# A causal seven-tap convolution ahead of two dense layers: part of the first tiles' taps moved from VectorE to TensorE as matmuls with diagonal matrices

## The reference, cut to what matters

```python
# x: (2, 4096, 192); weight: (8, 7); w_in: (192, 2048); w_out: (2048, 192), for both layers
w = softmax(weight, axis=-1)                                  # 8 heads of 24 channels, 7 taps
y[b, s, c] = sum_k w[head(c), k] * x_pad[b, s + k, c]         # causal: six zeros ahead of x
x = y.reshape(8192, 192)
h = x @ w_in1
P = a0 + a1*h + a2*h**2 + a3*h**3
Q = 1 + |b0|*|h| + |b1|*h**2
x = (P / (Q + 1e-6)) @ w_out1                                 # first layer: rational
h = x @ w_in2
out = (s * max(h, 0)**2 + b) @ w_out2                         # second layer: squared ReLU
```

## Time and profile before

| what | us |
|---|---|
| median of 3 runs | 1335.89 (1335.84 to 1336.78) |
| the profiled execution: its own time | 1336.83 |
| the profiled execution: span of its records | 1335.0 |
| PE busy | 1259.8 (94% of the span) |
| DVE busy | 1160.5 (87%) |
| ACT busy | 1098.3 (82%) |
| POOL busy | 333.9 (25%) |

### The profile page before, as it was taken

How to read it: one execution, slowest core, us unless ns; L and a number is a source line. 1 busy time by engine, 2 the same in 40 slices (tenths; PEclk the granted TensorE clock), 3 DMA queues, 4 the chain that set the end, 5 groups by cost and what they waited for, 6 DMA issues and landing times.

```text
span 1335.0 us, 16225 instructions
## 1 busy us (share of the span) xinstructions
PE 1259.8 (94%) x5920; PEld 1069.3 (80%) x5920; DVE 1160.5 (87%) x1073; ACT 1098.3 (82%) x1053; POOL 333.9 (25%) x145
## 2 busy tenths in 40 slices
PE   3665899999999999999999999999999999999998
PEld 2544688888888888888888888888888888888887
DVE  7999999998899989999899989999899998978810
ACT  4766788888888888888888888888898888888833
POOL 4233222222222222222222222222222222222200
PEclk9787899999999999999999999999999999999999
DMA  5310100001000100001000010001000000000000
GB/s 134 103 32 0 24 1 12 1 1 36 0 12 0 36 0 0 12 0 36 0 12 0 0 36 0 12 0 36 0 0 12 0 12 1 13 1 13 0 13 12
DMA packets 17885, 20.40 MB, mean 15 GB/s; under 512 B 1472, under 2 KB 13760, under 8 KB 17600
## 3 DMA queue, kind: packets, MB, share of 16 engines
q1 hardware_dynamic: 17712, 20.00, 5.5%
q10 hardware_dynamic: 144, 0.01, 0.0%
HBM read 13.72 MB, written 6.29 MB: 15 GB/s over the span
## 4 chain that ended last, share of the span: by engine, by line
PE 75%; DVE 12%; ACT 6%; issue 5%; POOL 0%; DVEq 0%; ACTq 0%
PE o L340 22%; PE h L314 7%; PE h L317 7%; PE h L315 7%; PE h L316 7%; PE h L318 7%; PE o_tail L329 3%; PE o L327 3%; PE o L328 3%; PE o_tail L331 3%; PE o L330 3%; DVE work L610 3%; DVE work L651 2%; DVE work L649 1%; DVE work L612 1%
## 5 line engine op out<-in xcount | busy, mean ns | idle before, releaser
L297 POOL TENSOR_TENSOR gl<-work,gh 128x1024 fp32r<-128x1024 f32 x128 | 309.1, 2415 | 913.2 <-ACT gh L477 913.2
L340 PE MATMUL o<-v,work 128*128 128x192 f32 x2048 | 355.8, 327 | 3.4 <-ACT work L492 3.4
L340 PEld LDWEIGHTS o<-v,work 128*128 128x128 f32 x2048 | 338.2, 190 | 20.9 <-ACT work L492 11.2
L314 PE MATMUL h<-x_hi,w_hi 128*128 128x512 f32 x512 | 226.5, 442 | 61.5 <-DVE work L615 40.6
L610 DVE SCALAR_TENSOR_TENSOR work<-work,coef,h 128x1024 f32<-128x1024 f32 x128 | 163.6, 1278 | 91.9 <-ACT work L470 91.9
L317 PE MATMUL h<-x_tail,w_tail_hi 128*128 128x512 f32 x512 | 206.6, 403 | 0.0
L315 PE MATMUL h<-x_lo,w_hi 128*128 128x512 f32 x512 | 206.3, 403 | 0.0
L468 ACT ACTIVATE work<-h,coef 128x1024 f32<-128x1024 f32 x128 | 153.9, 1203 | 63.2 <-PE h L318 58.1
L316 PE MATMUL h<-x_hi,w_lo 128*128 128x512 f32 x512 | 205.8, 402 | 0.0
L318 PE MATMUL h<-x_tail,w_tail_lo 128*128 128x512 f32 x512 | 204.6, 400 | 0.0
L480 ACT ACTIVATE work<-work 128x1024 f32<-128x1024 f32 x128 | 135.9, 1062 | 65.7 <-DVE work L610 63.9
(11 more groups left out here) (62 smaller groups left out, 1563.2 us busy)
## 6 DMA issues: line engine op xcount, KB each, us to landing
out_dram<-y_out SPq DMA_DIRECT2D x16, 384.0 KB, 2.6
xt<-in_x_main_dram SPq DMA_DIRECT2D x7, 518.0 KB, 4.7
xt_tail<-in_x_tail_dram SPq DMA_DIRECT2D x8, 259.0 KB, 5.4
work<-in_moe_w_out_dram SPq DMA_DIRECT2D x1, 1536.0 KB, 10.9
v<-in_moe_w_out_dram SPq DMA_DIRECT2D x1, 1536.0 KB, 7.2
work<-in_moe_w_in_dram SPq DMA_DIRECT2D x1, 1024.0 KB, 9.3
work<-in_moe_w_in_dram SPq DMA_DIRECT2D x2, 512.0 KB, 5.6
xt<-in_x_main_dram SPq DMA_DIRECT2D x2, 259.0 KB, 4.9
```

Of the source, the lines that this page charges most:

```text
L297: nc.gpsimd.tensor_tensor(gl[:, j % 2, :], r_buf[j % 2], gh[:, j % 2, :].bitcast(F32), ALU.subtract).then_inc(gl_ready, 1)
L314: pe.matmul(h[:, half, :], hi[:, c], x_hi[:, :], start=True, stop=False)
L340: last = pe.matmul(o2[:, c // 2, c % 2, 0:D], g, v2[:, f, :], start=(f == 0 and c % 2 == 0), stop=(f == FT - 1), skip_group_check=True)
```

## The change

Four of the first tile's seven main taps, all of the second tile's, and all of the second pair's (main channels of both batches and the tail) become matmuls on PE. Each tap is one full fp32 matmul of 512 columns with a 128x128 matrix that has the tap's weights on its diagonal, accumulated in a PSUM bank of `o2` that isn't used yet. POOL makes an identity, ACT scales it by a column of `cw` into the diagonals (seven for the main channels, seven more for the tail in the same memory later). ACT copies finished convolutions to SBUF (`copy_of_conv`) for tiles 1 to 3 and the tail; for the first tile DVE adds PE's part to its own three taps. ACT does tap 0 of the first tail. `CONV_AT` says in which unit PE takes which taps, always between its product for unit n + 1 and its second product for unit n - 3. The column sum goes from unit 4 to unit 3. `load_x(1)` waits for PE's second-tile taps in place of DVE's. w_out1 and w_out2 are laid out on the host by partition, so that each partition reads one run of 12 KB, and w_out1 is loaded ahead of the coefficients. Later pairs stay on DVE by `TAPS_AT`.

```diff
-    TAPS_AT_FIRST = {(0, 0): (("second", 0), ("second", 1)), (0, 1): (("second", 2), ("second", 3)),
-                     (0, 2): (("second", 4), ("second", 5)), (0, 3): (("second", 6),),
-                     (0, 6): (("pair", 0), ("tail", 0)), (0, 7): (("pair", 1), ("tail", 1)),
-                     (1, 0): (("pair", 2), ("tail", 2)), (1, 1): (("pair", 3), ("tail", 3)),
-                     (1, 3): (("pair", 4), ("tail", 4)), (1, 4): (("pair", 5), ("tail", 5)),
-                     (1, 5): (("pair", 6), ("tail", 6))}
+    PE_TAPS_OF_FIRST = (3, 4, 5, 6)
+    DVE_TAPS_OF_FIRST = (0, 1, 2)
+    CONV_AT = {0: (("second", (0, 1)),), 1: (("second", (2, 3)),), 2: (("second", (4, 5, 6)),),
+               4: (("pair_a", (0, 1, 2)),), 5: (("pair_a", (3, 4, 5)),),
+               6: (("pair_a", (6,)), ("pair_b", (0, 1))), 7: (("pair_b", (2, 3, 4)),), 8: (("pair_b", (5, 6)),),
+               10: (("tail", (0, 1, 2)),), 11: (("tail", (3, 4, 5, 6)),)}
...
+            sp.dma_start(raw_v1, w_out1).then_inc(v1_loaded, 16)
...
-                sp.wait_ge(main_step, counted(main_taps(pair - 1)))
-                sp.wait_ge(tail_step, counted(pair * TAPS))
+                sp.wait_ge(conv_summed, 2 if isinstance(pair, int) and pair == 1 else 5)
+                sp.wait_ge(tail_step, counted(tail_steps(pair - 1)))
...
+            nc.gpsimd.memset(ident, 0.0).then_inc(ident_ready, 1)
+            pool.wait_ge(ident_ready, 1)
+            nc.gpsimd.affine_select(out=ident, in_=ident, compare_op=ALU.not_equal, fill=1.0, base=0,
+                                    pattern=[[-1, P]], channel_multiplier=1).then_inc(ident_ready, 1)
...
+            def conv_taps(bank, rows, taps, first, last):
+                for k in taps:
+                    done = pe.matmul(conv_bank[bank], diag[k], rows[:, k:k + TOK], start=(k == first),
+                                     stop=(k == last))
+                if taps[-1] == last:
+                    done.then_inc(conv_summed, 1)
...
+                    if group == "tail":
+                        if starts:
+                            pe.wait_ge(diag_ready, 2 * TAPS)
+                            pe.wait_ge(conv_copied, 2)
+                        conv_taps(1, xt_tail[:, :], taps, 0, TAPS - 1)
...
+            pe.wait_ge(x0_loaded, 32)
+            for i, k in enumerate(PE_TAPS_OF_FIRST):
+                pe.wait_ge(diag_ready, i + 1)
+                conv_taps(0, xt[:, 0, :], (k,), PE_TAPS_OF_FIRST[0], PE_TAPS_OF_FIRST[-1])
...
-                    if j == 4 and first(t):
+                    if j == 3 and first(t):
...
+                    if early:
+                        conv_of_unit(n)
...
+            def diagonal(k, rows):
+                nc.scalar.activation(diag[k], ident, ACT.Identity, scale=cw[:, rows, k:k + 1]).then_inc(diag_ready, 1)
+            def copy_of_conv(dst, bank):
+                nc.scalar.copy(dst, conv_bank[bank]).then_inc(conv_copied, 1)
...
+            for k in PE_TAPS_OF_FIRST:
+                diagonal(k, 0)
+            act.wait_ge(x0_loaded, 32)
+            nc.scalar.activation(conv_tail[:, :], xt_tail[:, 0:TOK], ACT.Identity,
+                                 scale=cw[:, 1, 0:1]).then_inc(tail_step, 1)
             high_of_w1(0)
+            for k in DVE_TAPS_OF_FIRST:
+                diagonal(k, 0)
...
+                    if first(t) and j == 3:
+                        act.wait_ge(conv_summed, 2)
+                        copy_of_conv(conv[:, 1, :], 1)
+                    if first(t) and j == 7:
+                        act.wait_ge(conv_summed, 3)
+                        act.wait_ge(x1_lo_ready, 2)
+                        copy_of_conv(conv[:, 0, :], 1)
+                    if second(t) and j == 1:
+                        act.wait_ge(conv_summed, 4)
+                        for k in range(TAPS):
+                            diagonal(k, 1)
+                        act.wait_ge(x1_lo_ready, 4)
+                        copy_of_conv(conv[:, 1, :], 0)
+                    if second(t) and j == 4:
+                        act.wait_ge(conv_summed, 5)
+                        copy_of_conv(conv_tail[:, :], 1)
...
-            for k in range(TAPS):
+            for k in DVE_TAPS_OF_FIRST:
                 main_tap(slice(0, 1), k, 0, k)
-            for k in range(TAPS):
-                tail_tap(k, 0)
+            for k in range(1, TAPS):
+                tail_tap(k, 0, k)
+            dve.wait_ge(conv_summed, 1)
+            dve.wait_ge(main_step, len(DVE_TAPS_OF_FIRST))
+            nc.vector.tensor_tensor(conv[:, 0, :], conv_bank[0], conv[:, 0, :], ALU.add).then_inc(main_step, 1)
...
-                    if first(t) and j == 5:
+                    if first(t) and j == 4:
                         dve.wait_ge(colsum_ready, 1)
```

More of the change, by code:

```diff
@@ L130, in conv_rational_relu2_kernel @@
         y_out = sb("y_out", [P, SUB, D])
-        ones = y_out[:, 0, 0:P]
+        y_flat = y_out[:, :, :].rearrange("p c d -> p (c d)")
+        ones = y_flat[:, 0:P]
+        diag_more = sb("diag_more", [P, 3, P])
+        diag = [y_flat[:, (k + 1) * P:(k + 2) * P] for k in range(5)] + [diag_more[:, k, :] for k in range(2)]
+        ident = diag_more[:, 2, :]
         bias_row = sb("bias_row", [P, D])
@@ L146, in conv_rational_relu2_kernel @@
         o2 = psum("o2", [P, 2, 2, 256])
+        conv_bank = [o2[:, bank, :, :].rearrange("p a b -> p (a b)") for bank in range(2)]
         h1_flat = h1[:, :, :].rearrange("p a b -> p (a b)")
@@ L256, in phase @@
                     sp.wait_ge(w_lo_ready, 8)
[L257 removed]
+                    sp.dma_start(v2[:, :, :], w_out2).then_inc(v2_loaded, 16)
                     sp.wait_ge(v1_lo_ready, 2)
@@ L343, in second_product_2, with conv_of_unit @@
                 last.then_inc(out2_done, 1)
+            def conv_taps(bank, rows, taps, first, last):
[4 more added lines that the diff above has]
+                    done.then_inc(conv_summed, 1)
+            def conv_of_unit(n):
+                for group, taps in CONV_AT.get(n, ()):
+                    starts = taps[0] == 0
+                    if group == "second":
+                        if starts:
+                            pe.wait_ge(diag_ready, TAPS)
+                            pe.wait_ge(x0_second_loaded, 16)
+                        conv_taps(1, xt[:, 1, :], taps, 0, TAPS - 1)
+                    if group == "pair_a":
+                        if starts:
+                            pe.wait_ge(conv_copied, 1)
+                            pe.wait_ge(x_loaded, 32)
+                        conv_taps(1, xt[:, 0, :], taps, 0, TAPS - 1)
+                    if group == "pair_b":
+                        if starts:
+                            pe.wait_ge(bias_row_ready, 1)
+                        conv_taps(0, xt[:, 1, :], taps, 0, TAPS - 1)
+                    if group == "tail":
+                        if starts:
+                            pe.wait_ge(diag_ready, 2 * TAPS)
[5 more added lines that the diff above has]
+                conv_taps(0, xt[:, 0, :], (k,), PE_TAPS_OF_FIRST[0], PE_TAPS_OF_FIRST[-1])
             def product_of_layer_1(n, j, t, parity):
@@ L522, in tail_tap @@
                 else:
-                    dve.wait_ge(tail_step, counted(pair * TAPS + k))
+                    dve.wait_ge(tail_step, counted(step))
                     ins = nc.vector.scalar_tensor_tensor(dst, x_k, w_k, dst, ALU.mult, ALU.add)
@@ L530, in split_conv @@
                 done = pair * 2 + batch
-                dve.wait_ge(main_step, counted(TAPS if isinstance(done, int) and done == 0 else main_taps(pair)))
-                dve.wait_ge(tail_step, counted((pair + 1) * TAPS))
+                if isinstance(done, int) and done == 1:
+                    dve.wait_ge(conv_copied, 1)
+                else:
+                    dve.wait_ge(main_step, counted(main_steps(pair)))
+                    dve.wait_ge(tail_step, counted(tail_steps(pair)))
+                    if not isinstance(pair, int) or pair > 0:
+                        dve.wait_ge(conv_copied, 4)
                 dve.wait_ge(h1_ready, counted((done - 1) * UNITS))
@@ L634, in phase @@
                         split_conv(i, 1)
-                    for what, k in at(i, TAPS_AT, TAPS_AT_FIRST).get((parity, j), ()) if tile(t) else ():
-                        if what == "second":
-                            if k == 0:
-                                dve.wait_ge(x0_second_loaded, 16)
-                            main_tap(slice(1, 2), k, 0, TAPS + k)
-                        elif pair_exists(i + 1):
-                            if what == "pair":
-                                main_tap(slice(0, 2), k, i + 1, main_taps(i) + k)
-                            else:
-                                tail_tap(k, i + 1)
+                    convolves = tile(t) and pair_exists(i + 1) and not (first(t) or second(t))
+                    for what, k in TAPS_AT.get((parity, j), ()) if convolves else ():
+                        if what == "pair":
```

(6 more changed lines are left out.)

22 lines of the change are left out of this document (14 added, 8 removed).

## The result

The changed kernel takes 1320.64 us (median of four, 1320.41 to 1321.37) against 1335.87 for the kernel before: a ratio of 0.9886, 95% interval 0.9868 to 0.9903. The forecast was 1321.0, 14.8 us of gain against 15.2 of the medians. In the two profiled executions the span went from 1335.0 to 1319.0 us.

What follows compares the result with a forecast made beforehand. DVE was taken to bound the start (units 1 to 11) and TensorE the unchanged steady part. The terms 4.3 + 11.9 + 0.6 - 1.0 - 1.0 gave 14.8 us of gain, 1321.0 us against the median, range 1315 to 1328.

Steps and rivals of the forecast that it cites:

- part 1: Before unit 0: sharing the first tile's taps starts the first product earlier, gaining 4.3 us (3.0 to 5.3).
- part 2: Unit 0: no gain, since its two second-tile taps lie beside ACT's four casts, which set the chain.
- part 3: Units 1 to 11: taking pure tap time off DVE gains 11.9 us, with units left at 7.4 or so.
- part 5: TensorE's and ACT's new work: low-clock restarts make products late in units 4 (0.3) and 10 (0.7), -1.0 us (0 to -4.5).
- the two ends: Before unit 0: the first product's length, 2.4 us at full clock and 4.7 at the low clock.
- Part 4: POOL's subtractions beside DVE: unit 8 gains a net 0.6 us more, unit 9 gains 1.0 less than first counted.
- The rule that was quoted: Unit 9: two-SBUF-input VectorE and SBUF-reading GpSimd instructions exclude one another, first to issue goes first; sum 1.7 us less.
- warm rival: Start and unit 13: TensorE's clock doesn't fall with more matmuls between waits; gain about 19 us, 1317; chance 0.12.
- second rival: Units 4, 5 and 9: POOL and TensorE lag, unit 9 at 12.2 us; gain 9, total 1327; chance 0.20.
- slower rival: Units 2 to 11: TensorE at the low clock becomes the bound, 21 us slower, 1357; chance 0.05.
- The head start alone: Only the gain before unit 0 counts, as the ACT chain needs what DVE gave up: 4.3 us, 1331.5; chance 0.03.

Runs made afterwards that it cites:

- the combined kernel: Tail diagonals made early, POOL's second subtraction moved later and TensorE's first-tile taps repeated before the first product, all against the changed kernel: median 1317.62 us.

## Why the prediction was right

By its own terms, in us of gain, from the table of units:

| term | forecast | measured |
|---|---|---|
| part 1, before unit 0 | 4.3 | 3.3 |
| part 2, unit 0 | 0 | 0.1 |
| part 3, units 1, 2, 3, 6, 7, 11 | 8.1 | 8.3 |
| units 8 (parts 3 and 4) | 2.5 | 2.5 |
| unit 9 (parts 3 and 4) | 0.9 | 0.0 |
| unit 5 | 0 | 0.3 |
| part 5, units 4 and 10 | -1.0 | 0.0 |
| units 12 and 13 | 0 | 1.4 |
| sum | 14.8 | 15.9 |

**What bounds the start.** Right: DVE. Every unit without other work (1, 2, 3, 6, 7, 11) fell to 7.41 to 7.43, the 7.4 that was read off, and the chain through ACT did not take over. The steady units did not move.

**Part 1.** Right in its mechanism, short by 1.0. The split ended 0.2 us later than worked out; and the product took 4.2 us, not the 3.4 that lay between the two ends. Its price was sized wrongly, and the run with the repeated taps shows that the clock was the cause. The idle time it was read from was wrong too: TensorE's four taps took 5.4 us, not 6.9, so it stood idle for 4.36 us ahead of the product and not for 3.0. Taps that were faster than forecast, while DVE was the later one, were of no use and made the gap longer. Nor would 3.0 us have been safe: with the old layout the product began at the low clock behind 3.03 us, and in the run with nine more matmuls behind 2.93. A full fp32 tap at the high clock took 0.87 to 0.89 us as forecast.

**The layout.** Right: nothing, with 0.4 us as the most. The run gave 0.17 in the trace.

**Part 3.** Right to 0.2 us over six units. **Part 4.** Unit 8 right. Unit 9 is the term that was mis-sized: it took 11.44, between the 9.5 of one stretch and the 12.2 of two, and I had taken 10.5, nearer to one. Both stretches came. The rule that was quoted (the Trainium skill, SBUF — State Buffer, Who interferes with whom) was the better guide: each operation of DVE with two SBUF inputs that met a running subtraction waited for its end. The 12.2 overshot since a wait is 2.0 us, not a whole 2.4. Two runs show the mechanism: either edit that takes one meeting away takes 2.0 us off the unit, both together 4.0.

**Part 5.** Its lateness of TensorE did not show in units 4 and 10. For unit 10 the mechanism was right, but unit 9 hid it, by being longer than forecast: with unit 9 shorter by 2 us, DVE waited 0.62 and 0.67 us for TensorE in unit 10, against the 0.7 forecast, and with unit 9 shorter by 4 it waited 2.61. Two errors had hidden one another there. For unit 4 it was simply not late: DVE and ACT found the second product done.

**Units 12 and 13.** The step that failed is "taps in units 12 and 13 lie where TensorE's product is late anyway: nothing". The taps were indeed free (the run with idle work in unit 12), but the lateness itself went. TensorE's rows ahead of the two products concerned, before:

```profile
137.05 0.47 PE L314 MATMUL h<-x_hi,w_hi 128*128 128x512 f32 x1 [1.23 <-DVE work L615]
...
146.23 0.80 PE L314 MATMUL h<-x_hi,w_hi 128*128 128x512 f32 x1 [4.29 <-DVE work L615]
```

and after:

```profile
124.45 0.76 PE L336 MATMUL h<-x_hi,w_hi 128*128 128x512 f32 x1 [3.86 <-DVE work L713]
...
131.78 0.51 PE L336 MATMUL h<-x_hi,w_hi 128*128 128x512 f32 x1
```

Before, the product of unit 13 (146.23) came after a gap of 4.29 us and ran at the low clock. After, the low clock fell on the product ahead of it (124.45, 0.76 us for its first matmul), layer 2's first, which nobody waited for, and the one of unit 13 followed at 131.78 without a gap, at the high clock. Unit 12 became 1.75 us shorter, and unit 13 took 0.35 of that back. Five traces agree on the size: ACT's reading behind the product of unit 13 waited 1.70 us for TensorE in the kernel before, 0.89 and 0.72 where the clock fell within that product (idle work doubled, early diagonals), and not at all in the changed kernel and with the single idle work in unit 11, and unit 12 took 10.76, 9.95, 9.81, 9.01 and 8.98. The prediction had listed this as part of its warm rival.

**The rivals.** TensorE stayed warm in part: not at the start and not at the restarts in units 1, 6 and 9 (low clock from 35.47, 79.16 and 102.93 on), but for unit 13. POOL's lag came in unit 9 as one half of the second rival. The slower rival did not happen, but its mechanism is real: units 4 to 7 swallow 5.2 us more of TensorE's work for nothing, and of 15.7 us about half comes out. The head start alone is refuted by the table.

The two errors of about 1 us down (the start, unit 9) and the two up (lateness, unit 12) nearly cancelled. The total is nearer than its parts deserve: that it came within 1 us is luck. (The 15.9 of this table is against the traced execution before, which was 0.94 us above its median; by the medians the gain was 15.2.)

## What to carry to other kernels

Price a change in the ramp-up of a kernel unit by unit, by the distance between two starts of the same instruction, and take for each unit the largest of what its engines need; the terms here were right where one engine was full, and wrong where two engines had to meet. When work is moved off the bound engine, look at what each new instruction delays on its own engine, because that shifts the moment at which the next engine starts, and two engines that exclude each other may now overlap. And look for where TensorE's gaps of 3 to 4 us go: what costs is not the gap but which product is first behind it.

## What was not expected of the hardware

The length of a gap alone doesn't tell what follows. Behind gaps of 3.59 us (changed kernel, 101.84) and 4.01 us the product began at the high clock and fell during it, behind 3.91 and 3.86 it began at the low clock, and behind 2.10 and 2.41 it stayed high; but behind 2.44 (early diagonals, 129.53) it fell. At one and the same place, the restart in unit 1, behind 3.85 us in both, the run with the repeated taps began at the low clock (0.80 us for the first matmul) and the combined kernel at the high one (0.50). And in the run with nine more matmuls a gap of 2.93 us (at 17.55, behind the first taps of the kernel) was followed by the low clock, one of 2.95 (at 124.38, behind work at the high clock) by the high one, so what TensorE did before the gap may count too. One restart made unit 10 2.2 us longer in one version than in another; that this is why the executions of these two versions differ by 2.7 us, while those of the changed kernel stay within 1, fits, but no kernel has a second trace.

When the first small load landed differed too: DVE's first operation that waits for it started between 4.89 and 5.90 us over the traces here, and the start of unit 0 went with it, roughly (22.96 to 24.59 where the edit acts later). A single trace of a change in the start is no better than that.
